# A high/low split of q and k moved to GpSimd, and x's low product moved to VectorE

## The chip, the cores and the metric

The kernel runs on one core of one Trainium2 chip. The time is device microseconds (us) of one execution; the time before is the median of 3 runs. The engines are PE (TensorE; its weight loads are shown as PEld), DVE (VectorE), ACT (ScalarE), POOL (GpSimd) and SP (SyncE, which here only issues DMAs).

## The reference, cut to what matters

Three stages follow one another: causal attention with a cumulative bias, a feed-forward layer with `h - tanh(h)`, and a second feed-forward layer with softmax weighting and a layer norm.

```python
scores = scale * q @ k.T                       # q, k: (4, 8, 576, 64), float32
cum = np.cumsum(np.maximum(s, 0.0), axis=-1)
scores = np.where(causal, -1e9, scores + np.minimum(-(cum[..., :, None] - cum[..., None, :]), 0.0))
attn = softmax(scores)
x = (attn @ v)                                 # -> (2304, 512)
h = x @ w_in;   x = (h - np.tanh(h)) @ w_out   # 512 -> 2048 -> 512
h = x @ w2_in;  ...                            # 512 -> 1024, solu, layer norm, -> 512
```

The change touches the attention stage alone.

## The kernel before, in words

**High and low parts.** TensorE's operands here have the type float32r. Each operand is held as two float32r parts, high (a converted copy) and low (the operand minus its high part), and a product is made of three: high with high, high with low, low with high. Every operand that comes out of PSUM therefore takes two passes: ScalarE writes the high part with a Copy from PSUM, and VectorE reads the same PSUM bank again, subtracts the high part and writes the low part.

**Pairs and slots.** The 32 heads are taken as 16 pairs of heads. The attention stage is a software pipeline of slots, numbered s = -1 to 17; `attention()` writes the first five and the last four out and runs slots 4 to 13 in a loop, two at a time. In slot s each engine works on several pairs at once, through closures that look up `sl.pair(k)`:

- k = 1, the pair s+1: its q and k are turned by TensorE (transposes with an identity) and split. `turn_qk(n)` (L1299 to L1302) turns part n into PSUM: n = 0 is the 64-row tail of k and q (192 columns), n = 1 the 512 columns of q, n = 2 the 512 columns of k. All three use one bank, `qk_ps`, so each must be read out before the next is turned. ScalarE's `qk_copy(n)` (L717) writes the high part and VectorE's `qk_rest(n)` (L994) the low part; `turn_qk(n)` waits for `qk_lo`, that is for VectorE, before it writes the bank again.
- k = 0, the pair s: scores (`score`, L1211 and L1215 for the mask; `score_tail`, L1229, L1231), VectorE's `bias` (L963, which also gives the row's maximum), ScalarE's `exp` (L707). The first matmul of `score(0, 1)` waits until all parts of q and k of this pair are split. GpSimd's `sums` (L537, L540) copies the tail's cumulative sums, and `split_v` (L568, L570) splits v into high and low.
- k = -1, the pair s-1: its probabilities are turned in seven units A01, A2, A3, T, B01, B2, B3 (`turn_p`, L1283), read out by ScalarE (`p_hi`, L698) and VectorE (`p_lo`, L946) in that order. The units share two banks in turn, so that TensorE writes a unit only when the unit two before it has its low part. `turn_rden` (L1311) and `rden_rows_copy` (L725) turn the reciprocal denominators; SP then writes them to memory and later reads them back, spread over the partitions. `attend(-1, 0, ...)` (L1254) multiplies the first head's probabilities with v.
- k = -2, the pair s-2: `attend(-2, 1, ...)` does the second head. One attend gives high products in 64 partitions of PSUM and low products in the other 64. ScalarE's `x_low_part(h)` (L732) copies the low product to the partitions of the high one, in SBUF; VectorE's `x_add(h)` (L976) adds the two into `x_sum`; GpSimd's `scale_x` (L557) multiplies with the reciprocal denominators into `xT`. `x_low_part(0)` and `x_add(0)` stand at the start of a slot, `x_low_part(1)` and `x_add(1)` in its middle.

**What sets the order.** Each engine runs its own instruction list in the order written at the end of its `slot` function; engines meet only at counting semaphores. TensorE's list in a slot is: score(0, 1), A01, A2, turn_qk(0), score(2), attend(-2, 1, 0), A3, turn_rden, the rest of attend(-2, 1), T, turn_qk(1), score(3), B01, B2, turn_qk(2), attend(-1, 0, 0), score_tail, attend(-1, 0, 1), B3, the rest of attend(-1, 0). SP's list is, too, one queue: in a slot it loads the next cumulative sums and v, then waits for `rden_rows`, writes the denominators out, and only behind that loads q and k of the pair s+2, whose parts `turn_qk` of the next slot needs.

From slot 15 on the first layer's work is woven in: `first_x` (L637 on ScalarE, L887 on VectorE) and `first_w1i` split x and weights, `first_up` is its matmuls.

Of the kernel before, what the change touches and what calls it, by code (L numbers as in the profile page):

```python
# [14 lines left out]
P = 128  # L15
# [35 lines left out]
def build_transformer(nc, q, k, v, s, w_in, w_out, w2_in, w2_out, g_ln, out):  # L51
# [59 lines left out]
    with ctx:  # L111
# [12 lines left out]
        with ExitStack() as phase:  # L124
            sb = tensors(phase, attention_words)
            qkT_hi = [sb(f"qkT_hi{n}", [P, QK_W], F32R) for n in range(2)]
            qkT_lo = [sb(f"qkT_lo{n}", [P, QK_W], F32R) for n in range(2)]
            probs = [sb(f"probs{n}", [P, PW]) for n in range(2)]
            pT_hi = sb("pT_hi", [P, 2, PT_W], F32R)

            v_parts = [sb(f"v_parts{n}", [P, NT, 4 * D], F32R) for n in range(2)]
            ident_b = sb("ident_b", [P, P], BF16)
            mask_b = sb("mask_b", [P, P], BF16)
            upper_b = sb("upper_b", [P, TAIL], BF16)
            lower_b = sb("lower_b", [P, TAIL], BF16)
            tail_mask_b = sb("tail_mask_b", [P, TAIL], BF16)
            neg_max = [sb(f"neg_max{n}", [P, TILES]) for n in range(2)]
            row_sum = [sb(f"row_sum{n}", [P, TILES]) for n in range(2)]
            den = [sb(f"den{n}", [P, TILES]) for n in range(2)]
            rden = [sb(f"rden{n}", [P, TILES]) for n in range(2)]  # L140
            rden_row = sb("rden_row", [TILES, P])

            w1i_words = GATE_W + FT * 2 * DM
            sb("gap", [P, w1i_words - sum(attention_words)])
            cum_bc = [sb(f"cum_bc{n}", [P, 2, S]) for n in range(2)]
            cum_tail = sb("cum_tail", [P, S])
            v_raw = [sb(f"v_raw{n}", [P, NT, 2 * D]) for n in range(2)]
            pT_lo = sb("pT_lo", [P, 2, PT_W], F32R)
            rden_T = [sb(f"rden_T{n}", [P, S]) for n in range(2)]
            x_low = sb("x_low", [P, S])  # L150
            x_sum = sb("x_sum", [P, S])
# [96 lines left out]
        cum_copied = sem("cum_copied")  # L248
        qk_hi = sem("qk_hi")
# [248 lines left out]
        def _(pool):  # L498
# [28 lines left out]
            def slot(sl):  # L527
                def sums():

                    if sl.runs(0):  # L530
                        pair, half, par = sl.pair(0)
                        pool.wait_ge(cum_in[par], 16 * (half + 1))
                        wait(pool, biased, TILES * pair)
                        wait(pool, v_split, 2 * pair)
                        wait(pool, x_done, pair - 2)
                        met(pool)
                        pool.tensor_copy(cum_tail[0:TAIL, :], cum_bc[par][0:TAIL, 0, :]).then_inc(cum_copied, 1)  # L537
                        pool.wait_ge(cum_copied, 2 * pair + 1)
                        met(pool)
                        pool.tensor_copy(cum_tail[TAIL:P, :], cum_bc[par][TAIL:P, 1, :]).then_inc(cum_copied, 1)  # L540

                def scale_x():
                    if sl.runs(-2):
# [7 lines left out]
                        if sl.runs(0):  # L551
                            pool.wait_ge(cum_copied, 2 * sl.pair(0)[0] + 2)
                        else:
                            pool.wait_ge(x_done, pair)
# [4 lines left out]
                def split_v():  # L559
                    if sl.runs(0):  # L560
# [3 lines left out]
                        pool.wait_ge(cum_copied, 2 * pair + 2)  # L564
                        wait(pool, x_done, pair - 1)
# [3 lines left out]
                        pool.wait_ge(v_split, 2 * pair + 1)  # L569
                        pool.tensor_tensor(low(v_parts[par]), raw, high(v_parts[par]).bitcast(F32),  # L570
                                           ALU.subtract).then_inc(v_split, 1)

                sums()
                scale_x()
# [50 lines left out]
        def _(act):  # L625
# [65 lines left out]
            def slot(sl):  # L691
# [19 lines left out]
                def qk_copy(n):  # L711

                    if sl.runs(1):
# [3 lines left out]
                        act.activation(qkT_hi[par][:, at:at + width], qk_bank(sl, n)[:, 0:width], ACT.Copy).then_inc(qk_hi, 1)  # L717
# [8 lines left out]

                def x_low_part(h):

                    if sl.runs(-2):
                        pair, half, par = sl.pair(-2)  # L730
                        act.wait_ge(attended, 2 * pair + h + 1)
                        act.activation(x_low[h * D:(h + 1) * D, :], x_ps[(1 - h) * D:(2 - h) * D, :],  # L732
                                       ACT.Copy).then_inc(x_low_done, 1)
# [14 lines left out]
                x_low_part(0)  # L748
# [10 lines left out]
                p_hi("A3")  # L759
                rden_rows_copy()  # L760
# [6 lines left out]
                x_low_part(1)  # L767
                p_hi("T")
                first_w1i(sl, 1)
                qk_copy(1)  # L770
# [5 lines left out]
                qk_copy(2)  # L776
# [88 lines left out]
        def _(dve):  # L865
# [73 lines left out]
            def slot(sl):  # L939
# [28 lines left out]

                def x_add(h):
# [18 lines left out]
                def qk_rest(n):  # L988

                    if sl.runs(1):  # L990
                        pair, half, par = sl.pair(1)
                        at, width = QK_PART[n]
                        dve.wait_ge(qk_hi, 3 * pair + n + 1)
# [3 lines left out]
                if sl.fixed and sl.s == 0:  # L997
# [12 lines left out]
                    return  # L1010
                bias(0, 0)
# [10 lines left out]
                qk_rest(0)  # L1022
# [3 lines left out]
                if sl.fixed and sl.s == LAST:  # L1026
                    step(0, 0)
                x_add(1)
                p_lo("T")
                first_w1i(sl, 1)  # L1030
                qk_rest(1)
# [5 lines left out]
                qk_rest(2)  # L1037
# [100 lines left out]
        def _(pe):  # L1138
# [58 lines left out]
            def slot(sl):  # L1197
# [88 lines left out]
                def turn_qk(n):  # L1286

                    if sl.runs(1):
# [6 lines left out]
                        else:  # L1295
                            wait(pe, qk_lo, 3 * pair + n)
# [31 lines left out]
                turn_p("A3")  # L1328
                turn_rden()
                attend(-2, 1, 1, 2, 3, 4)  # L1330
                turn_p("T")
                turn_qk(1)
# [5 lines left out]
                turn_qk(2)  # L1338
# [104 lines left out]
```

## Time and profile before

| what | us |
|---|---|
| median of 3 runs (lowest to highest) | 840.17 (839.23 to 841.72) |
| the profiled execution | 841.88 |
| its span, from the first to the last instruction | 840.1 |
| attention, slots -1 to 17 | about 0 to 232 |
| one slot of the loop, from one first bias to the next (120.65 to 133.13) | 12.48 |

The granted TensorE clock is 0.996 of full speed over the span. Busy shares over the whole span are PE 98%, DVE 54%, ACT 47%, POOL 15%, but the last three are averages over stages with different limits; in the attention stage VectorE and ScalarE are busy more than nine tenths of a slot. In the rows, a duration contains the time in which an instruction's end overlaps the next one's start: what an instruction takes from its engine is the distance from its start to the next start. A bracket at the end of a row gives how long the engine sat idle before it and who released it. In the chain of waits, "issue" is time in which the engine waited for nothing that the profile shows.

### The profile page before, as it was taken

Reading aid. Unit: us, or ns where it says so; the run is one execution under the profiler, and the core shown is the slowest. Engines: PE = TensorE matmul, PEld = TensorE weight load, DVE = VectorE, ACT = ScalarE, POOL = GpSimd, SP = SyncE. Lnnn points to the kernel's source line nnn. Section 1 sums busy time; section 2 is a strip of 40 time slices with the busy share of each in tenths; the row PEclk is TensorE's granted clock in tenths of the full one; section 3 lists DMA queues with packets and bytes.
Section 4 is the critical chain, followed back from the end, with each engine's and each line's share of the span. In section 5 each row is a group of like instructions: output and inputs, shape, how many; then the busy total and the mean of one; then the engine's idle time right before and its main releaser. Section 6 shows DMA issues by size and latency. Waiting matters only on the chain.

```text
span 840.1 us, 14119 instructions
## 1 busy us (share of the span) xinstructions
PE 821.1 (98%) x4552; PEld 706.4 (84%) x4552; DVE 452.4 (54%) x1059; ACT 395.1 (47%) x888; POOL 126.6 (15%) x150
## 2 busy tenths in 40 slices
PE   7999999998999999999999999999999999999998
PEld 6787787787888888888888888899988888888886
DVE  5889999988764342223223322333647554555452
ACT  4999999998744332223222322324533433333323
POOL 3334334334100000000000000000022212221110
PEclk9999999999999999999999999999999999999999
DMA  7454554554343200000000000000200100000001
GB/s 179 130 152 121 149 154 127 142 155 132 90 158 106 76 0 1 1 1 0 0 0 0 0 0 0 0 1 26 76 0 2 38 12 25 25 25 12 25 25 38
DMA packets 77714, 46.29 MB, mean 55 GB/s; under 512 B 59824, under 2 KB 68144, under 8 KB 77680
## 3 DMA queue, kind: packets, MB, share of 16 engines
q1 hardware_dynamic: 75232, 45.19, 18.9%
q10 hardware_dynamic: 2448, 0.66, 0.4%
q8 instruction: 19, 0.31, 0.2%
q14 instruction: 15, 0.12, 0.0%
HBM read 40.97 MB, written 4.87 MB: 55 GB/s over the span
## 4 chain that ended last, share of the span: by engine, by line
PE 82%; DVE 6%; issue 5%; ACT 4%; SPq 1%; DMA 1%; DVEq 0%; ACTq 0%
PE psum L1156 24%; PE psum L1169 24%; PE psum L1367 12%; PE psum L1395 11%; PE psum L1254 4%; ACT probs L707 2%; PE psum L1381 2%; PE psum L1211 2%; DVE pT_lo L946 2%; PE psum L1229 1%; PE psum L1283 1%; ACT x_low L732 1%; PE psum L1299 1%; DVE qkT_lo L994 1%; DVE probs L963 1%
## 5 line engine op out<-in xcount | busy, mean ns | idle before, releaser
L1156 PE MATMUL psum<-x_hi,w1i 128*128 128x464 f32 (+1 forms) x640 | 185.7, 371 | 0.4 <-DVE w1i L892 0.4
L1169 PE MATMUL psum<-gate_hi,w1o 128*128 128x464 f32 (+1 forms) x640 | 146.5, 371 | 0.0
L1156 PEld LDWEIGHTS psum<-x_hi,w1i 128*128 128x128 f32 x640 | 119.8, 188 | 14.8 <-DVE w1i L892 0.8
L1169 PEld LDWEIGHTS psum<-gate_hi,w1o 128*128 128x128 f32 x640 | 120.1, 188 | 13.6
L926 DVE TENSOR_TENSOR gate_lo<-gate,gate_hi 128x464 fp32r<-128x464 f32 (+1 forms) x80 | 51.1, 639 | 135.8 <-ACT gate_hi L677 135.8
L1156 PE MATMUL psum<-x_lo,w1i 128*128 128x464 f32 (+1 forms) x320 | 118.8, 371 | 0.0
L677 ACT ACTIVATE gate_hi<-gate 128x464 fp32r<-128x464 f32 (+1 forms) x80 | 47.1, 589 | 144.7 <-PE psum L1169 137.8
L916 DVE TENSOR_TENSOR gate<-psum,gate 128x464 f32<-128x464 f32 (+1 forms) x80 | 50.9, 636 | 97.3 <-ACT gate L666 97.2
L666 ACT ACTIVATE gate<-psum 128x464 f32<-128x464 f32 (+1 forms) x80 | 44.2, 553 | 107.2 <-PE psum L1156 104.5
L1395 PE MATMUL psum<-w2o,lnT_hi 128*128 128x512 f32 x288 | 91.8, 400 | 0.5 <-DVE lnT_lo L1112 0.5
L707 ACT ACTIVATE probs<-probs,neg_max 128x128 f32<-128x128 f32 (+2 forms) x144 | 83.7, 582 | 13.6 <-DVE neg_max L963 13.0
L1169 PE MATMUL psum<-gate_lo,w1o 128*128 128x464 f32 (+1 forms) x320 | 80.0, 371 | 0.0
L1367 PE MATMUL psum<-w2i,y_hi 128*128 128x512 f32 x288 | 77.4, 391 | 0.0
L946 DVE TENSOR_TENSOR pT_lo<-psum,pT_hi 128x512 fp32r<-128x512 f32 (+3 forms) x160 | 72.1, 479 | 4.1 <-ACT pT_hi L698 3.5
L698 ACT ACTIVATE pT_hi<-psum 128x512 fp32r<-128x512 f32 (+3 forms) x160 | 64.2, 437 | 11.2 <-PE psum L1283 9.2
L591 POOL CAST y_hi<-xT 128x512 fp32r (+1 forms) x18 | 11.0, 612 | 387.6 <-PE psum L1156 384.2
L963 DVE CUSTOM_DVE_ANT_0 probs<-psum,cum_bc 128x128 f32<-128x128 f32 (+3 forms) x128 | 58.8, 482 | 16.5 <-PE psum L1215 12.4
L1156 PEld LDWEIGHTS psum<-x_lo,w1i 128*128 128x128 f32 x320 | 60.1, 188 | 6.7
L1169 PEld LDWEIGHTS psum<-gate_lo,w1o 128*128 128x128 f32 x320 | 60.1, 188 | 6.5
L1283 PE MATMUL psum<-ident,probs 128*128 128x128 f32 x400 | 61.2, 278 | 3.0 <-DVE pT_lo L946 1.6
L1367 PEld LDWEIGHTS psum<-w2i,y_hi 128*128 128x128 f32 x288 | 54.0, 188 | 11.8 <-issue 0.2
L1395 PEld LDWEIGHTS psum<-w2o,lnT_hi 128*128 128x128 f32 x288 | 52.9, 189 | 11.9 <-issue 1.0
(109 smaller groups left out, 1226.0 us busy)
## 6 DMA issues: line engine op xcount, KB each, us to landing
cum_bc<-cum_dram SPq DMA_DIRECT2D x16, 576.0 KB, 5.0
rden_T<-rden_dram SPq DMA_DIRECT2D x32, 144.0 KB, 3.0
out_x<-out_sb SPq DMA_DIRECT2D x18, 256.0 KB, 2.0
stage<-in_q SPq DMA_DIRECT2D x32, 128.0 KB, 2.3
v_raw<-in_v SPq DMA_DIRECT2D x32, 128.0 KB, 3.6
stage<-in_moe_w_in SPq DMA_DIRECT2D x16, 256.0 KB, 3.0
stage<-in_moe_w_out SPq DMA_DIRECT2D x16, 256.0 KB, 3.1
stage<-in_k SPq DMA_DIRECT2D x28, 128.0 KB, 2.4
```

The lines of the kernel that those rows point to most:

```text
L677: act.activation(gate_hi[j % 2][:, 0:wide(c)], gate[j % 2][:, 0:wide(c)], ACT.Copy).then_inc(gate_hi_done, 1)
L698: hi = act.activation(to(pT_hi), ps, ACT.Copy)
L707: act.activation(probs[par][:, at:at + width], probs[par][:, at:at + width], ACT.Exp, bias=neg_max[par][:, col:col + 1], scale=-1.0, accum ...
L916: dve.tensor_tensor(gate[j % 2][:, 0:n], h_ps[j % 4][:, 0:n], gate[j % 2][:, 0:n], ALU.subtract).then_inc(gate_done, 1)
L926: dve.tensor_tensor(gate_lo[j % 2][:, 0:n], gate[j % 2][:, 0:n], gate_hi[j % 2][:, 0:n].bitcast(F32), ALU.subtract).then_inc(gate_lo_done, 1)
L946: lo = dve.tensor_tensor(to(pT_lo), ps, to(pT_hi).bitcast(F32), ALU.subtract)
L963: dve.tensor_tensor_reduce(probs[par][:, at:at + width], tail_bank(sl) if h is None else score_ps[h][t], cum_tail[:, :] if h is None else ...
L1156: mm = pe.matmul(h_ps[j % 4][:, 0:wide(c)], wp[j][:, kt, :], xp[:, kt, 0:wide(c)], start=(n == 0), stop=(n == 3 * KT - 1))
L1169: mm = pe.matmul(y_ps[m][:, 0:wide(c)], wp[j][:, m * P:(m + 1) * P], gp[j % 2][:, 0:wide(c)], start=(j == 0 and wp is w1o_hi and gp is gat ...
L1283: mm = pe.transpose(ps[:, n * P:(n + 1) * P], probs[par][:, at:at + P], ident[:, :])
L1367: mm = pe.matmul(h2_ps[par][:, half * BANK:(half + 1) * BANK], yp[par][:, kt, :], wp[kt][:, 4 * half:4 * half + 4, :].rearrange("q f p -> ...
L1395: mm = pe.matmul(out_ps[par], lp[par][:, f, :], wp[f][:, :], start=(f == 0 and n == 0), stop=(f == FT2 - 1 and n == 2))
```

## The change

Splitting q and k: for pairs 2 to 15 ScalarE's `qk_copy(n)` now writes a plain float32 copy of the turned part into one of two new SBUF buffers, `qk_flat[n % 2]`, and signals `qk_copied`. GpSimd's new `split_qk(n)` makes both parts from that buffer, a cast for the high and a subtraction for the low part. VectorE's `qk_rest` is left only for pairs 0 and 1 (slots -1 and 0). `turn_qk(n)` on TensorE now waits for ScalarE's copy, not for the low part. ScalarE's `qk_copy(0)` and `qk_copy(2)` wait for GpSimd to be done with the buffer that they reuse.

The low product of x: `x_low_part(h)` is a VectorE copy in place of a ScalarE one; its second half also waits for `rden_rows` of the slot.

Order: TensorE's `turn_qk(1)` moves ahead of `turn_rden` and of the rest of attend(-2, 1), `turn_qk(2)` moves from behind B2 to behind T; `qk_copy(1)` and `qk_copy(2)` move up on ScalarE in the same way. On GpSimd `split_qk` 0 to 2 stand between `sums` and `scale_x`.

```diff
+            qk_flat = [sb(f"qk_flat{n}", [P, FULL * P]) for n in range(2)]
...
@@ GpSimd
-                        wait(pool, x_done, pair - 2)
...
+                def split_qk(n):
+
+                    if sl.runs(1) and not (sl.fixed and sl.s <= 0):
+                        pair, half, par = sl.pair(1)
+                        at, width = QK_PART[n]
+                        flat = qk_flat[n % 2][:, 0:width]
+                        hi, lo = qkT_hi[par][:, at:at + width], qkT_lo[par][:, at:at + width]
+                        pool.wait_ge(qk_copied, 3 * pair + n + 1)
+                        if n == 0:
+                            pool.wait_ge(cum_copied, 2 * (pair - 1) + 2)
+                        else:
+                            pool.wait_ge(qk_lo, 3 * pair + n)
+                        met(pool)
+                        pool.tensor_copy(hi, flat).then_inc(qk_hi, 1)
+                        pool.wait_ge(qk_hi, 3 * (pair - 2) + n + 1)
+                        met(pool)
+                        pool.tensor_tensor(lo, flat, hi.bitcast(F32), ALU.subtract).then_inc(qk_lo, 1)
...
                 sums()
+                split_qk(0)
+                split_qk(1)
+                split_qk(2)
                 scale_x()
                 split_v()
...
@@ ScalarE
-                        act.activation(qkT_hi[par][:, at:at + width], qk_bank(sl, n)[:, 0:width], ACT.Copy).then_inc(qk_hi, 1)
+
+                        if sl.fixed and sl.s <= 0:
+                            to = qkT_hi[par][:, at:at + width]
+                        else:
+                            to = qk_flat[n % 2][:, 0:width]
+                            if n != 1:
+                                act.wait_ge(qk_lo, 3 * pair + (n == 2))
+                        act.activation(to, qk_bank(sl, n)[:, 0:width], ACT.Copy).then_inc(qk_copied, 1)
...
-                x_low_part(0)
...
                 p_hi("A3")
+                qk_copy(1)
                 rden_rows_copy()
                 exp(0, 2)
...
-                x_low_part(1)
                 p_hi("T")
                 first_w1i(sl, 1)
-                qk_copy(1)
+                qk_copy(2)
...
-                qk_copy(2)
...
@@ VectorE
+                def x_low_part(h):
+
+                    if sl.runs(-2):
+                        pair, half, par = sl.pair(-2)
+                        dve.wait_ge(attended, 2 * pair + h + 1)
+                        if h == 1 and sl.runs(-1):
+
+                            dve.wait_ge(rden_rows, pair + 2)
+                        dve.tensor_copy(x_low[h * D:(h + 1) * D, :], x_ps[(1 - h) * D:(2 - h) * D, :]).then_inc(x_low_done, 1)
...
+                x_low_part(0)
                 bias(0, 0)
                 bias(0, 1)
                 x_add(0)
...
-                qk_rest(0)
...
+                x_low_part(1)
                 x_add(1)
                 p_lo("T")
                 first_w1i(sl, 1)
-                qk_rest(1)
...
-                qk_rest(2)
...
@@ TensorE
-                            wait(pe, qk_lo, 3 * pair + n)
+                            wait(pe, qk_copied, 3 * pair + n)
...
                 turn_p("A3")
+                turn_qk(1)
                 turn_rden()
                 attend(-2, 1, 1, 2, 3, 4)
                 turn_p("T")
-                turn_qk(1)
+                turn_qk(2)
...
                 turn_p("B01")
                 turn_p("B2")
-                turn_qk(2)
                 attend(-1, 0, 0)
```

## Rows read from the trace of the kernel before

**Rows 1.** Busy time by stretch (PE, PEld, DVE, ACT, POOL), one slot of the loop

```profile
core 0: us, PE busy (x) PEld busy (x) DVE busy (x) ACT busy (x) POOL busy (x), PEclk, DMA share, GB/s
120.65:133.13 12.48, 12.30 (x102) 10.09 (x101) 11.45 (x35) 11.55 (x34) 5.03 (x5) 1.00 0.57 145
```

**Rows 2.** Chain of waits, same slot: start, us, what

```profile
120.65 0.11 DVE probs L963
...
122.75 0.04 ACT probs L707
...
127.28 0.69 DVE qkT_lo L994
...
128.02 0.66 PE psum L1299 x4
...
133.13 0.11 DVE probs L963
```

**Rows 3.** VectorE's timeline, same slot: start, duration, instruction

```profile
122.44 0.27 DVE L963 CUSTOM_DVE_ANT_0 probs<-psum,cum_bc 128x128 f32<-128x128 f32 x1
...
124.98 0.68 DVE L946 TENSOR_TENSOR pT_lo<-psum,pT_hi 128x512 fp32r<-128x512 f32 x1
125.88 0.76 DVE L976 TENSOR_TENSOR x_sum<-psum,x_low 64x576 f32<-64x576 f32 x1 [0.23 <-ACT x_low L732]
126.67 0.69 DVE L946 TENSOR_TENSOR pT_lo<-psum,pT_hi 128x512 fp32r<-128x512 f32 x1
...
131.22 1.21 DVE L946 TENSOR_TENSOR pT_lo<-psum,pT_hi 128x384 fp32r<-128x384 f32 x2
```

**Rows 4.** ScalarE's timeline, same slot

```profile
123.64 0.30 ACT L717 ACTIVATE qkT_hi<-psum 128x192 fp32r<-128x192 f32 x1
...
124.33 0.25 ACT L725 ACTIVATE rden_row<-psum 9x128 f32<-9x128 f32 x1
```

**Rows 5.** TensorE's timeline, same slot (short matmuls overlap; x4 is four of them)

```profile
122.91 0.60 PE L1283 MATMUL psum<-ident,probs 128*128 128x128 f32 x4
...
123.48 0.45 PE L1254 MATMUL psum<-pT_hi,v_parts 128*128 128x448 f32 x1
...
124.52 0.28 PE L1254 MATMUL psum<-pT_lo,v_parts 128*128 128x64 f32 x1
124.63 0.66 PE L1283 MATMUL psum<-ident,probs 128*128 128x128 f32 x4
...
125.70 0.50 PE L1211 MATMUL psum<-qkT_hi 64*128 64x512 f32 x2
...
126.72 1.25 PE L1283 MATMUL psum<-ident,probs 128*128 128x128 f32 x7
...
128.43 0.56 PE L1254 MATMUL psum<-pT_hi,v_parts 128*128 128x128 f32 x2
```

**Rows 6.** Groups of instructions, whole span, shapes kept apart

```profile
L994 DVE TENSOR_TENSOR qkT_lo<-psum,qkT_hi 128x512 fp32r<-128x512 f32 x32 | 21.9, 686 | 1.1 <-ACT qkT_hi L717 0.7
...
L1049 DVE COPY xT<-psum 128x464 f32 x4 | 2.4, 636 | 3.2 <-PE psum L1169 3.2
```

**Rows 7.** Groups of GpSimd, whole span, shapes kept apart

```profile
L594 POOL TENSOR_TENSOR y_lo<-xT,y_hi 128x512 fp32r<-128x512 f32 x18 | 23.3, 1295 | 3.3 <-POOL y_hi L591 3.3
...
L591 POOL CAST y_hi<-xT 128x512 fp32r x14 | 8.6, 612 | 0.0
```

**Rows 8.** VectorE's timeline in slot 15, L887

```profile
200.01 0.64 DVE L887 TENSOR_TENSOR x_lo<-xT,x_hi 128x464 fp32r<-128x464 f32 x1
202.89 1.55 DVE L887 TENSOR_TENSOR x_lo<-xT,x_hi 128x464 fp32r<-128x464 f32 x1
```

**Rows 9.** GpSimd's timeline in slot 15

```profile
202.52 1.42 POOL L557 TENSOR_TENSOR xT<-x_sum,rden_T 128x576 f32<-128x576 f32 x1 [6.84 <-DVE x_sum L976]
```

**Rows 10.** SP's queue, the slot of rows 1: start, issue time

```profile
130.52 0.65 SPq L395 DMA_DIRECT2D stage<-in_k  x1
```

**Rows 11.** DMA view, the same slot: last column us from issue to landing

```profile
stage<-in_k SPq DMA_DIRECT2D x1, 32.0 KB, 2.2
```

More of the change, by code:

```diff
@@ L248, in build_transformer @@
         cum_copied = sem("cum_copied")
+        qk_copied = sem("qk_copied")
         qk_hi = sem("qk_hi")
@@ L550, in scale_x @@
                         pool.wait_ge(rden_in[par], 32 * (half + 1))
-                        if sl.runs(0):
+                        if sl.runs(1):
+                            pool.wait_ge(qk_lo, 3 * sl.pair(1)[0] + 3)
+                        elif sl.runs(0):
                             pool.wait_ge(cum_copied, 2 * sl.pair(0)[0] + 2)
@@ L564, in split_v @@
                         pool.wait_ge(cum_copied, 2 * pair + 2)
+                        if sl.runs(1) and not (sl.fixed and sl.s <= 0):
+                            pool.wait_ge(qk_lo, 3 * sl.pair(1)[0] + 3)
                         wait(pool, x_done, pair - 1)
@@ L569, in split_v @@
                         pool.wait_ge(v_split, 2 * pair + 1)
+                        met(pool)
                         pool.tensor_tensor(low(v_parts[par]), raw, high(v_parts[par]).bitcast(F32),
@@ L725, in rden_rows_copy @@
                         act.activation(rden_row[:, :], rden_ps, ACT.Copy).then_inc(rden_rows, 1)
[L727 to L733, printed above, removed]
                 if sl.fixed and sl.s == 0:
@@ L992, in qk_rest @@
                         at, width = QK_PART[n]
-                        dve.wait_ge(qk_hi, 3 * pair + n + 1)
+                        dve.wait_ge(qk_copied, 3 * pair + n + 1)
                         dve.tensor_tensor(qkT_lo[par][:, at:at + width], qk_bank(sl, n)[:, 0:width],
@@ L1010, in slot @@
                     return
+                if sl.fixed and sl.s < 0:
+                    for n in range(3):
+                        qk_rest(n)
+                    return
+                x_low_part(0)
                 bias(0, 0)
```

## The prediction

> **What bounds the kernel now.** I began with the busy times of one slot [rows 1]. Of 12.48 us VectorE works 11.45 and ScalarE 11.55, GpSimd only 5.03: two engines are nearly full, and the one that gets work has room. A nearly full engine is no proof of a bound, so I read the chain of waits next [rows 2]. It closes in one slot: the slot's first bias at 120.65, a hand-over to ScalarE at 122.75, VectorE's low part of q at 127.28, which lets TensorE turn k at 128.02, and then TensorE alone up to the next first bias at 133.13. A slot is thus 7.37 us of alternating engines and 5.11 us of TensorE. Below, an offset is a time minus 120.65; the question is where the next first bias comes to lie.
>
> **What is removed and what is added.** VectorE loses three subtractions a slot: the two of 512 columns take 0.60 each from start to next start (686 ns with the overlap [rows 6]; p_lo(T), as wide, is followed after 0.61 [rows 2, 3]), the short one about 0.3. It gets two copies of 64x576 out of PSUM. No such copy is in the trace. Two rows bound it: VectorE's PSUM copy of 464 columns takes 636 ns [rows 6], and a 64x576 addition out of PSUM takes 0.76 [rows 3]. I take 0.75, and 0.64 and 0.76 as ends. So VectorE's load hardly changes (minus 1.5, plus 1.5). ScalarE loses two copies, and that is a real relief. GpSimd gets three casts and three subtractions: 512 columns cost 612 and 1295 ns [rows 7]; for the 192 columns I scale these down to an estimated 0.3 and 0.5. With an estimated 0.15 of waiting before each of the six this is about 5.5 us, so GpSimd stands at 10.5 to 11.7 of 12.5. It has no chain of its own: walked through, it begins when the first copy is there (offset 3.3), ends the last subtraction near 9.0, and the scores of the next slot need it at 11.1. The scaling of x and the split of v follow to about 13.3, and the sums and the next split fit before 15.9. I charge nothing for GpSimd; if that cover went, each us beyond two would lengthen the slot.
>
> **The early q turn.** Here the order matters. turn_qk(1) now stands behind A3. A3 starts at 122.91 [rows 5]; four transposes take 0.41 from start to next start (128.02 to 128.43 [rows 2, 5]), so TensorE comes to turn_qk(1) at offset 2.67. The bank is free when ScalarE has copied part 0, and that copy starts at 123.64 and takes 0.30 [rows 4]: offset 3.29, with the hand-over 3.37. Can the relieved ScalarE make it earlier? No: in front of it are two exps that begin at 122.75, released by VectorE's bias of 122.44 [rows 2, 3], and VectorE has no gap before that bias. So TensorE stands still for 0.70 in the place of shorter waits later.
>
> From 3.37 TensorE alone gives a lower bound. turn_qk(1) 0.41, the denominators 0.04 (estimated), the rest of attend(-2, 1) from 123.48 to 124.63, 1.15: T begins at 4.97. T 0.44 and turn_qk(2) with the change to the scores 0.57: score(3) at 5.98. score(3) from 125.70 to 126.72, 1.02: B01 at 7.00. Seven transposes at 0.11: attend(-1, 0, 0) at 7.77. From 128.43 to the next first bias are 4.70 [rows 2, 5]. Sum: 12.47, the slot of today.
>
> **The low product.** attend(-2, 1) ends 1.32 after its second part began (124.52 plus 0.28 minus 123.48 [rows 5]): at 3.82 plus 1.32, 5.14. VectorE is waiting by then, since even where it stands today p_lo(A3) ends at 5.01 [rows 3]. x_low_part(1) runs 5.18 to 5.93, x_add(1) 5.96 to 6.72, p_lo(T) 6.75 to 7.44. Today p_lo(T) ends at 6.71. B2 needs its bank: 7.49, so attend(-1, 0, 0) at 7.82 instead of 7.77, and TensorE's part ends at 12.52.
>
> x_low_part(0) stands at the end of the same stretch. The last p_lo (B3) ends at 132.43 [rows 3], 4.00 after attend(-1, 0, 0), because ScalarE must first read B3: here 11.82, and 0.05 later since ScalarE's exps are queued behind a later B01. x_low_part(0) runs 11.90 to 12.65 and the first bias begins at 12.68. VectorE, not the masks of TensorE, is then late, by 0.16. Slot: 12.68 against 12.48, plus 0.20.
>
> In this I let each of the four changes of partition wait for the instruction in front. The trace shows why: after x_add(1), on the upper 64 partitions, the next instruction starts 0.79 later, after its 0.76 have ended, whereas p_lo(T) is followed 0.61 after its start though it takes 0.69 [rows 3]. The Trainium skill (VectorE: DVE Perf Modes, "Two Vector instructions with no wait between them") says the same as a model: an instruction whose input or output starts in another quarter of the partitions than the last one's is held until all earlier ones have finished. By it both new copies and what follows them are held; without it the slot would be 12.5. The trace agrees with the rule.
>
> A second rule speaks against the change. In slot 15 a subtraction of 0.64 took 1.55 while GpSimd worked from 202.52 on [rows 8, 9]. Both its inputs are in SBUF. VectorE's instructions in slots 1 to 14 have one input in PSUM, and p_lo(T) or the subtraction at 127.28 are not longer beside GpSimd (0.69, 0.69) than p_lo(A3) without it (0.68 [rows 2, 3]). So I charge nothing. The Trainium skill (SBUF — State Buffer, "Who interferes with whom") draws this same line: only an instruction with two SBUF inputs, or in a two-port mode, contends with GpSimd. By the rule the cost is zero in these slots; the trace agrees.
>
> **The ends.** Slots 2 to 14 have both parts of the change: 13 times 0.20 is 2.6. Slot 1 has no x; by the same walk it loses about 0.3. Slot 15 splits no q and k, so VectorE only gets work: x_low_part(1) behind p_lo(A3) instead of beside it, about 0.55. Slots 16 and 17 hide most of it behind the first layer's matmuls; about 0.3 stays in the last one. Sum: 2.6 minus 0.3 plus 0.55 plus 0.3, about 3.1. The profiled execution took 841.88 (span 840.1 and 1.8 around it), so 845.0 by it; it was 1.71 above the median, so 843.3 against 840.17.
>
> **Rivals.** (a) No change: TensorE alone bounds the slot and the copies of x stay in its shadow. That is the 12.47 above; it holds if the holds or the 0.75 are smaller by 0.16 in all. With the ends, plus 0.5: 840.7. For it: the margin is small. Against: the row after x_add(1). 0.34.
> (b) Faster: ScalarE, relieved of its copies, has part 0 in SBUF by offset 2.67, and turn_qk(1) doesn't stand. Then TensorE's bound falls to 11.8, and VectorE's chain decides: x_low_part(1) at 5.04, p_lo(T) ends 7.30, slot 12.5 by rows and at best 12.25 with cheap copies. 13 times minus 0.23 plus 0.5 is minus 2.5 or better: 837.6. It decides only if the bias of 122.44 comes 0.6 earlier, for which I see no source. 0.13.
> (c) Slower by more: q and k arrive late. rden_rows_copy now stands behind qk_copy(1), which waits for the early turn: it starts at 4.50 instead of 3.68 [rows 4]. SP's loads are queued behind it. The last load of k is issued at 9.87 and lands 2.2 later, at 12.07 [rows 10, 11]; 0.8 later is 12.9, and turn_qk(0) wants it at 12.99. Nothing is left in reserve; if it comes 0.5 late in each slot, half of it behind the wait for the second bias, 3 to 4 us come on top: 847. 0.08.
> (d) The engines' contention does reach instructions with one SBUF input: then the 0.9 of slot 15 comes once or twice a slot, 13 to 25 us, 855 to 868. 0.03.
> My forecast, plus 3.1, has 0.42.
>
> **How the numbers follow.** A difference of 0.3%, 2.5 us, is about what a measurement of this kernel can tell from no change. The forecast's own range is 840.7 to 846 (a slot by 0 to 0.4 longer), and it holds the bound of 842.7, so a good part of it counts as no change. Same: 0.13 from the forecast, 0.27 from (a), 0.01 from (b), 0.41. Faster: 0.12 from (b), 0.02 from (a), 0.14. Slower: the rest, 0.45. The range goes from 837.6, which takes in the better half of (b), to 847.5, past (c), and leaves (d) out.
>
> **What would show it.** Right: VectorE's p_lo(T) at offset 6.75 and later; turn_qk(1) with some 0.6 idle in front, released by ScalarE's copy; x_low_part(1) waiting for TensorE; the first bias directly behind x_low_part(0) without a gap; no stall of the scores on GpSimd. Wrong: an idle VectorE before the first bias (then (a)); part 0 copied before 3.0 (then (b)); TensorE waiting for in_k (then (c)); subtractions on VectorE above 0.7 (then (d)).

## The result, and the profile after

The changed kernel took 844.33 us (median of 7 runs, 843.95 to 846.71) against 840.17 for the kernel before (7 runs, 839.23 to 841.95): ratio 1.0049, 95% interval 1.0034 to 1.0064. It is slower by half a per cent. The forecast was 843.3 and "slower" by a little.

I cut each profiled span at four places: the first bias of slot 2, the first bias of slot 15, the first matmul of the first layer that waits for w1i behind the attention stage ("first_up" in the tables), and the end. "Slots" is the distance between the first two, over 13.

| profile | slot 2 begins | slots 2 to 14, mean | slot 15 to first_up | rest |
|---|---|---|---|---|
| before | 32.61 | 12.567 | 36.08 | 608.04 |
| after | 31.95 | 12.762 | 39.02 | 608.02 |
| difference | -0.66 | +0.195 (x13 = 2.54) | +2.94 | -0.02 |

Now the slot of the loop that answers to rows 1 to 5. First the busy time by stretch, from one first bias to the next (PE, PEld, DVE, ACT, POOL):

```profile
121.25:134.00 12.75, 12.21 (x101) 10.12 (x100) 11.99 (x35) 10.35 (x33) 9.79 (x12) 1.00 0.55 139
```

Against [rows 1], ScalarE lost 1.2 us, GpSimd got 4.8 and VectorE is fuller than before: 11.99 of 12.75. Its own load was to stay the same. It rose by 0.5, and the timeline of VectorE shows where:

```profile
123.56 0.64 DVE L1018 TENSOR_SCALAR den<-row_sum 128x9 f32<-128x9 f32 x1
...
125.76 0.69 DVE L970 TENSOR_TENSOR pT_lo<-psum,pT_hi 128x512 fp32r<-128x512 f32 x1
126.48 0.75 DVE L1001 COPY x_low<-psum 64x576 f32<-64x576 f32 x1
127.27 0.76 DVE L1010 TENSOR_TENSOR x_sum<-psum,x_low 64x576 f32<-64x576 f32 x1
128.06 0.69 DVE L970 TENSOR_TENSOR pT_lo<-psum,pT_hi 128x512 fp32r<-128x512 f32 x1
...
132.49 0.69 DVE L970 TENSOR_TENSOR pT_lo<-psum,pT_hi 128x512 fp32r<-128x512 f32 x1 [0.22 <-ACT pT_hi L725]
133.21 0.76 DVE L1001 COPY x_low<-psum 64x576 f32<-64x576 f32 x1
134.00 0.29 DVE L987 CUSTOM_DVE_ANT_0 probs<-psum,cum_bc 128x128 f32<-128x128 f32 x1
```

The first row is the operation on the denominators, over 128x9 elements. It takes 0.64 here, and took 0.16 before, as the groups of instructions of the kernel before show:

```profile
L984 DVE TENSOR_SCALAR den<-row_sum 128x9 f32<-128x9 f32 x16 | 2.5, 159 | 0.0
```

One thing differs from the walk: x_low_part(1) doesn't wait for TensorE. It follows p_lo(A3) directly, since the longer operation makes VectorE late. The rest is as walked through: the copy takes 0.75; p_lo(T) starts 6.81 after the slot's first bias (6.75 was forecast); the last p_lo, the copy and the next first bias follow each other 0.72 and 0.79 apart, each start waiting for the end in front.

The chain of waits of the same slot:

```profile
121.25 0.14 DVE probs L987
...
124.31 0.22 ACT qk_flat L751
124.54 0.04 issue
124.58 0.66 PE psum L1336 x4
...
133.29 0.33 PE psum L1252 x4
133.62 0.35 PE psum L1320 x3
133.97 0.03 issue
134.00 0.29 DVE probs L987
```

turn_qk(1) is L1336: released by ScalarE's copy at offset 3.33 (3.37 was forecast). From there the chain as drawn runs on TensorE to the end. But the masks of the scores (L1252) are done at 133.62, while the first bias starts at 134.00, behind a VectorE copy that ends at 133.97. In the kernel xlow_scalar below, where no copy stands there, the bias follows 0.18 after the masks. So VectorE is late by about 0.20 (134.00 against 133.80); 0.16 was forecast.

TensorE's timeline has the stand before the early q turn. The bracket counts 0.50 from the end of A3; counted as I had counted, 0.41 behind A3's start, it is 0.69, and 0.70 was forecast:

```profile
123.48 0.60 PE L1320 MATMUL psum<-ident,probs 128*128 128x128 f32 x4
124.58 0.66 PE L1336 MATMUL psum<-ident,stage 128*128 128x128 f32 x4 [0.50 <-ACT qk_flat L751]
```

GpSimd's timeline, at the same time:

```profile
123.51 0.67 POOL L541 COPY cum_tail<-cum_bc 64x576 f32<-64x576 f32 x1 [0.16 <-POOL cum_tail L538]
124.77 0.34 POOL L556 CAST qkT_hi<-qk_flat 128x192 fp32r<-128x192 f32 x1 [0.60 <-ACT qk_flat L751]
125.30 0.60 POOL L559 TENSOR_TENSOR qkT_lo<-qk_flat,qkT_hi 128x192 fp32r<-128x192 f32 x1 [0.18 <-POOL qkT_hi L556]
...
129.10 1.29 POOL L559 TENSOR_TENSOR qkT_lo<-qk_flat,qkT_hi 128x512 fp32r<-128x512 f32 x1 [0.18 <-POOL qkT_hi L556]
131.03 1.42 POOL L578 TENSOR_TENSOR xT<-x_sum,rden_T 128x576 f32 x1 [0.64 <-POOL qkT_lo L559]
```

It waits for another engine once, 0.60 before the first cast; all its other gaps stand behind its own instructions. The last low part ends at offset 9.14, and the next slot's scores take it without a wait. So it is hidden, but without that one wait its queue would still need 12.1 us (12.75 less 0.60) for a slot.

The ends hold the surprise. The busy time by stretch of the changed kernel, in slot 16 (the column after the counts of GpSimd is the granted clock):

```profile
212.00:214.00 2.00, 0.85 (x6) 0.64 (x6) 1.94 (x4) 1.32 (x5) 0.00 (x0) 1.00 0.56 214
214.00:216.00 2.00, 1.88 (x8) 1.71 (x9) 1.97 (x8) 1.14 (x3) 0.00 (x0) 0.58 0.00 0
216.00:218.00 2.00, 2.00 (x11) 1.84 (x9) 1.19 (x2) 0.74 (x2) 0.00 (x0) 0.57 0.00 0
```

TensorE was busy 0.85 of the first 2 us, and then its granted clock fell to 1.2 GHz for most of the next 4, in which it had nothing but matmuls to do. From attend(-2, 1, 0) of slot 16 to the first layer's next matmul TensorE took 4.36, where it took 2.76 before at 2.4 GHz. That alone is 1.60 of the 2.94.

### The profile page after: what moved, and what is told of

The parts are those of the page before. It is cut to its first block, busy times and chain, and to the rows that moved or that the text cites. A ratio compares the mean times of both kernels' runs of the same rounds, so it can differ in the third digit from the quotient of the medians.

```text
span 844.9 us, 14328 instructions
## 1 busy us (share of the span) xinstructions
PE 820.2 (97%) x4552; PEld 707.7 (84%) x4552; DVE 461.7 (55%) x1049; ACT 375.6 (44%) x856; POOL 192.8 (23%) x234
## 4 chain that ended last, share of the span: by engine, by line
PE 84%; DVE 5%; issue 4%; ACT 3%; SPq 1%; DMA 1%; DVEq 0%; ACTq 0%
PE psum L1206 23%; PE psum L1193 23%; PE psum L1404 12%; PE psum L1432 11%; PE psum L1291 3%; PE psum L1320 3%; PE psum L1248 2%; PE psum L1418 2%; PE psum L1336 2%; DVE probs L987 1%; DVE pT_lo L970 1%; ACT pT_hi L725 1%; ACT probs L734 1%; PE psum L1266 1%; DVE x_low L1001 1%
```

## The experiments

All comparisons are against runs of the kernel before on the same chip (medians 840.57, 840.81 and 841.80 in the three sets of runs).

**The low product on VectorE, alone.** The kernel before with only `x_low_part` moved.

```diff
@@ ScalarE
-                x_low_part(0)
-                x_low_part(1)
@@ VectorE
+                x_low_part(0)
                 bias(0, 0)
...
+                x_low_part(1)
                 x_add(1)
```

> The kernel before with one part of the change: x_low_part on VectorE; q and k are split and turned as before. My theory (the two copies lie on VectorE's chain: p_lo(T) is pushed out by about 0.6, turn_qk(2) and attend(-1, 0, 0) follow it, and x_low_part(0) stands between the last p_lo and the first bias): a slot of 13.0 to 13.3 us against 12.57 on average before, 6 to 9 us in 13 slots, and the ends of the attention stage about 3 us longer as in the changed kernel; 849 to 852. Rival (VectorE's load is what counts, and 1.5 us fit in its gaps of 1.0 us): about 13.1 too, but with no idle time left on VectorE at all. Rival (the copies are hidden): 840.

850.37, ratio 1.0116 (1.0099 to 1.0133); slots 13.158. The two copies cost 0.59 a slot while VectorE still splits q and k. They stand on the chain of waits ("DVE x_low L967"). The relief for ScalarE does not make up for them.

**The split and the new order, without the copies.** The changed kernel with `x_low_part` back on ScalarE.

```diff
@@ VectorE
-                x_low_part(0)
-                x_low_part(1)
@@ ScalarE
+                x_low_part(0)
                 p_hi("A01")
...
+                x_low_part(1)
                 p_hi("T")
```

> The changed kernel with x_low_part back on ScalarE at its old places; GpSimd splits q and k, and the q and k turns stand early. My theory: the early turn of q still waits for ScalarE's first copy, so TensorE alone gives 12.5, and p_lo(T) still ends near 7.5 because x_low_part(1) comes late; without a copy before the first bias the slot is 12.50 to 12.60 (12.76 in the changed kernel), and the ends are as before: 839.5 to 840.5. Rival (GpSimd's work or its contention made the slot longer): it stays at 12.75, 842. Rival (the copies of x cost nothing in the slot): 12.75 too.

843.23, ratio 1.0028 (1.0018 to 1.0038); slots 12.717, seven of them 12.64 to 12.67; the longest are slot 2 with 12.88 and slot 5 with 12.87, in which TensorE also waits 0.79 for the load of k. My expectation missed by 3 us. The chain of this kernel measures TensorE alone:

```profile
123.31 0.32 ACT qk_flat L751
123.63 0.04 issue
123.68 0.66 PE psum L1334 x4
...
132.44 0.34 PE psum L1250 x4
132.84 0.13 issue
132.96 0.11 DVE probs L997
```

turn_qk(1) at offset 3.36, then 9.28 us of TensorE to the next first bias. I had summed 9.10 from distances between starts. So TensorE by itself gives 12.64, not 12.47 (12.55 by the changed kernel's masks, which end at 133.62, plus the same 0.18). Even without the copies the change lengthens the slot of 12.57. Rival (a) would have come out slower than I said.

**The old order of the turns.** The changed kernel, with `turn_qk(1)`, `turn_qk(2)` and the two ScalarE copies where they stood before.

```diff
                 turn_p("A3")
-                turn_qk(1)
                 turn_rden()
...
                 turn_p("T")
-                turn_qk(2)
+                turn_qk(1)
...
                 turn_p("B2")
+                turn_qk(2)
```

> The changed kernel with the old order of the turns (turn_qk(1) behind T, turn_qk(2) behind B2, ScalarE's copies with them); x_low_part stays on VectorE. If the early order is the fault, as 0.70 us of standing in front of turn_qk(1) may suggest: 12.5 or less, 840. My theory says otherwise: without the early turn attend(-2, 1) ends earlier, but VectorE reaches x_low_part(1) only at 5.2, p_lo(T) ends at 7.5 all the same, and now turn_qk(2) stands between B2 and attend(-1, 0, 0), 0.4 more; GpSimd gets part 2 later, and all it does moves towards the next slot: 13.0 to 13.3 a slot, 847 to 851.

853.91, ratio 1.0159 (1.0141 to 1.0176); slots 13.539, the later ones 13.65. That is 3 us slower than I expected. The early turns are not an extra: fed later, GpSimd ends its last low part late and the next scores wait for it, and TensorE's matmuls wait up to 0.7 for the denominators (its weight loads up to 1.0).

**The split alone.** GpSimd splits; the copies on ScalarE, the order as before (both edits above together).

> Only the split on GpSimd: x_low_part on ScalarE, all turns in the old order. VectorE has 1.5 us less to do and nothing more. My theory: p_lo(T) ends near 6.65, TensorE comes to attend(-1, 0, 0) at 7.45, a slot of 12.15 by TensorE; but part 2 reaches GpSimd only at about 8.7 and is ready near 11, so the scores of the next slot wait some tenths: 12.3 to 12.5, 836.5 to 839. Rival (GpSimd, with 12.1 us a slot in the changed kernel, becomes the bound and pushes itself on from slot to slot): 12.6 to 13, 841 to 846.

848.98, ratio 1.0095 (1.0074 to 1.0115); slots 13.158. I expected this one to be faster, and that theory fell. The rival came true in its effect, a longer slot, but not as it was put: GpSimd doesn't push itself on from slot to slot, since it still waits about 1.3 us in each for ScalarE's copies (0.96 and 0.32 in the slot shown). It is its delay that stands on the chain of waits:

```profile
119.10 0.50 ACT qk_flat L751
...
119.80 0.61 POOL qkT_hi L556
...
120.58 1.28 POOL qkT_lo L559
...
121.99 0.96 PE psum L1246 x12
...
125.87 0.88 DVE den L1018
```

k leaves PSUM at 119.1 to 119.6, and the first scores start 2.4 us later because cast and subtraction take 0.61 and 1.29 on GpSimd. And then the small operation on the denominators is on the chain with 0.88. Beside it, in the timelines of VectorE and GpSimd:

```profile
125.80 0.94 DVE L1018 TENSOR_SCALAR den<-row_sum 128x9 f32<-128x9 f32 x1
...
125.16 1.55 POOL L594 TENSOR_TENSOR v_parts<-v_raw,v_parts 128x640 fp32r<-128x640 f32 x1 [0.18 <-POOL v_parts L591]
```

It ends at 126.74, 0.03 after GpSimd's subtraction of v (126.71).

**The sums later.** The changed kernel with GpSimd's `sums()` behind `split_qk(0)`, and with the semaphore waits to match.

```diff
-                sums()
                 split_qk(0)
+                sums()
                 split_qk(1)
```

> The changed kernel with GpSimd's two copies of the sums behind the first split instead of in front of it, so that they no longer run while VectorE works on its small den operation. If GpSimd's work in SBUF holds that operation up (0.16 before, 0.61 to 0.64 after), it is back at 0.16 here. Then x_low_part(1) waits for TensorE as I had forecast, at an offset of 5.2, and the slot hardly gets shorter: 12.70 to 12.74, 843.7 to 844.3. A rival that takes this delay for the cause of the longer slot says 0.3 to 0.4 less a slot, 12.35 to 12.45 and 839 to 840.

844.71 (843.7 to 847.1), ratio 1.004 (1.0028 to 1.0051); slots 12.795, of which one is 13.11 and most are 12.74 to 12.77. The operation on the denominators met no copy of the sums any more, but in ten slots it met the subtraction of v and took 0.22 to 0.47 instead of the 0.16 that I expected; in the other three it took 0.16. x_low_part(1) waits for TensorE again (0.20). The slot stays: this delay, up to 0.5 us in ten slots of the changed kernel, costs nothing there, since x_low_part(1) has to wait for TensorE anyway. The changed kernel's own slots 4 and 7 say the same: there the operation took 0.16, and slot 7 is no shorter (12.74) than those around it.

**The low product left out.** The copies of x read and write the same partitions; the true low product isn't added. Everything else is as in the changed kernel.

```diff
-                        dve.tensor_copy(x_low[h * D:(h + 1) * D, :], x_ps[(1 - h) * D:(2 - h) * D, :])
+                        dve.tensor_copy(x_low[h * D:(h + 1) * D, :], x_ps[h * D:(h + 1) * D, :])
```

> The changed kernel, but x_low_part copies within the partitions in which the source lies (the high product in place of the low one), so that input and output start in the same partitions. It leaves out the low product of x. Everything else, the waits too, stays. If a change of partition holds the next instruction: what follows p_lo(B3), x_low_part(0) and p_lo(A3) starts about 0.08 before the end of the one in front in some of these places, 0.1 to 0.2 a slot in all; with TensorE's own chain at 12.64 the slot comes down to 12.64 to 12.68. Rival (the holds are nothing but waits on semaphores): no start changes, 12.75.

843.22 in its single run; slots 12.639, the steady ones 12.57. VectorE's timeline before a first bias:

```profile
131.59 0.69 DVE L970 TENSOR_TENSOR pT_lo<-psum,pT_hi 128x512 fp32r<-128x512 f32 x1 [0.21 <-ACT pT_hi L725]
132.20 0.74 DVE L1001 COPY x_low<-psum 64x576 f32<-64x576 f32 x1
132.91 0.29 DVE L987 CUSTOM_DVE_ANT_0 probs<-psum,cum_bc 128x128 f32<-128x128 f32 x1
```

The copy starts 0.61 after p_lo instead of 0.72, before that has ended, and the bias 0.71 after the copy instead of 0.79. The first change of partitions costs 0.11. The second costs at least 0.08, and how much more can't be seen, because the bias now stands 0.18 behind the masks and so is TensorE's again:

```profile
132.39 0.34 PE psum L1252 x4
```

Without them the slot is 0.12 to 0.17 shorter. The operation on the denominators takes 0.16 in nine slots of this run, which the run above shows to be worth nothing. The Trainium skill (VectorE: DVE Perf Modes, "Two Vector instructions with no wait between them") has as a rule that such an instruction starts only when every earlier one has finished; the runs agree.

**q and k loaded before the denominators.** In the changed kernel SP issues the loads of q and k ahead of its wait for `rden_rows`.

```diff
@@ SP, in the slot
+                if sl.runs(2) and not (sl.fixed and sl.s < 0):
+                    ...
+                    load_qk(pair, par)
                 if sl.runs(-1):
                     sp.wait_ge(rden_rows, pair + 1)
```

> The changed kernel with SP's queue turned round in a slot: q and k of the pair s+2 are loaded before SP waits for rden_rows. In the changed kernel TensorE waits 2.7 us in seven slots for in_k, and in more of them something unseen. My theory (VectorE decides the first bias, so these waits are taken up before score(2)): the waits for in_k vanish, the slot stays at 12.72 to 12.76, 844. Rival (the late loads of q and k are the cause of the longer slot): 12.6 or less, 842.

845.24, ratio 1.0049 (1.0034 to 1.0065); slots 12.756, as the changed kernel. TensorE's waits for in_k, 2.7 us in seven times in the changed kernel, are gone, and nothing is gained. Rival (c) came true as a wait and was worth nothing. The wait lies behind the first bias, before score(2), and something later in the slot takes it up; what does was not taken apart.

**The ends with the copies on ScalarE.** The changed kernel with `x_low_part` on ScalarE from slot 15 on.

```diff
@@ ScalarE
+                    if sl.runs(-2) and sl.fixed and sl.s >= PAIRS - 1:
@@ VectorE
-                    if sl.runs(-2):
+                    if sl.runs(-2) and not (sl.fixed and sl.s >= PAIRS - 1):
```

> The changed kernel, but in slots 15 to 17 x_low_part is on ScalarE again, as before; slots 2 to 14 are the changed ones. In the changed kernel the way from slot 15's first bias to the first full chunk of the first layer took 39.0 us against 36.1 before, 2.9 longer; 1.6 of these lie in slot 16, where the granted clock fell to 0.5 a second time behind TensorE's waits. My theory (VectorE's copies hold TensorE up in slots 15 and 16, and the waits bring the clock down): 36.2 to 36.6, no second stretch at half clock, 841.5 to 842 (844.3 changed). Rival (the second stretch is an accident of one profiled execution): it may be there again, and the time falls by 1 at most. Rival (the ends are paid by GpSimd's later work or later loads): 39 us as before, 844.

843.85 (842.3 to 846.26), ratio 1.0036 (1.0024 to 1.0047), 2 us above what I expected. The ends took 35.18, with the clock at 2.4 GHz throughout, but the start of this profile, with the same code, was 1.5 longer than that of the changed kernel (slot 2 begins at 33.42), with 6.8 us at 1.2 GHz in it instead of 3.4. The size of the ends' cost needed a fairer pair:

**Both kernels once more, unaltered.**

> The changed kernel once more, unaltered, for one profile: does TensorE's second stretch at half speed, during slot 16, come again? If it is bound to the changed kernel's work there, it stands again at 213 to 218 us and the way from slot 15's first bias to the end of slot 16 takes 39 us. If it hangs on small differences from run to run, it is gone and that way takes 36.5 to 37.5. The slots 2 to 14 give 12.74 to 12.78 either way.

> The kernel before once more, unaltered, for one profile, to price the way from slot 15's first bias to the end of slot 16 without the clock's part in it. With one stretch of 3.4 us at half speed it was 36.08. If the clock stays up here, 35.0 to 35.4, so that VectorE's copies of x cost 1.1 to 1.5 there (after_again: 36.50 with the clock up). If the same stretch comes again it is 36.0 to 36.2 and this comparison stays open but for ends_scalar (35.18). Slots 2 to 14 keep 12.57 on average.

844.50 and 841.47. In both the clock stays up through slots 15 and 16. The stretches of after_again that answer to those shown above:

```profile
212.00:214.00 2.00, 1.37 (x10) 1.12 (x10) 1.96 (x5) 1.48 (x5) 0.00 (x0) 1.00 0.68 259
214.00:216.00 2.00, 2.00 (x18) 1.94 (x17) 1.97 (x5) 1.19 (x3) 0.00 (x0) 1.00 0.03 12
216.00:218.00 2.00, 2.00 (x13) 1.81 (x12) 1.92 (x3) 1.12 (x2) 0.00 (x0) 1.00 0.01 2
```

| profile | slot 2 begins | slots 2 to 14, mean | slot 15 to first_up | rest |
|---|---|---|---|---|
| before_again | 33.20 | 12.566 | 35.07 | 608.07 |
| after_again | 32.17 | 12.766 | 36.50 | 608.07 |
| difference | -1.03 | +0.200 (x13 = 2.60) | +1.43 | 0.00 |

So of the 2.94 in the first pair 1.43 stays with the clock up, and 1.5 goes with the clock, which fell twice in the profile after and once in the one before (36.08 against 35.07). The 1.43 belongs to the copies of x, but for 0.11: ends_scalar, which has them back on ScalarE, takes 35.18, 0.11 more than before_again.

Laid over each other from slot 15's first bias on, TensorE's timelines of the two kernels show where it arises. TensorE is 0.66 late behind slot 15's x_low_part(1), 1.04 late at attend(-2, 1, 0) of slot 16, and 1.43 at the last point. In ends_scalar the three are 0.00, 0.12 and 0.11. The second place, in before_again and in after_again:

```profile
210.83 0.58 PE L1254 MATMUL psum<-pT_hi,v_parts 128*128 128x128 f32 x2 [0.35 <-DVE x_sum L976]
```

```profile
213.44 0.58 PE L1291 MATMUL psum<-pT_hi,v_parts 128*128 128x128 f32 x2 [0.63 <-DVE x_sum L1010]
```

**q alone on GpSimd.** The kernel before; ScalarE copies q plainly, GpSimd splits it behind `scale_x`; the tail and k stay with ScalarE and VectorE, and so do the copies of x and the order.

```diff
@@ GpSimd
                 scale_x()
+                split_q()
                 split_v()
@@ ScalarE, qk_copy
+                        if n == 1 and not (sl.fixed and sl.s <= 0):
+                            to = q_flat[:, :]
@@ VectorE, qk_rest
-                    if sl.runs(1):
+                    if sl.runs(1) and not (n == 1 and late):
@@ TensorE, turn_qk
+                        elif n == 2:
+                            wait(pe, qk_hi, 3 * pair + n)
```

> A version built from the readings: the kernel before, in which GpSimd splits part 1 alone, the 512 columns of q, from ScalarE's plain copy; parts 0 and 2 stay with ScalarE and VectorE, x_low_part stays on ScalarE, all turns stay in the old order; turn_qk(2) waits for the copy of part 1 instead of its low part. It takes 0.60 out of the one place where VectorE stood on the chain of waits (p_lo(T), then the low part of q, then turn_qk(2)), and gives GpSimd 2.2 us, placed behind scale_x so that VectorE's small den instruction isn't met. My theory: attend(-1, 0, 0) 0.3 earlier, a slot of 12.2 to 12.35 against 12.57, 836 to 838.5. Rival (ScalarE, busy 11.55 a slot, or TensorE is the next bound at once): 12.45 to 12.57, 839 to 840.5.

837.83 (10 runs, 837.44 to 840.09), ratio 0.997 (0.996 to 0.998); slots 12.348. Faster than both, at the weak end of what I expected. Its chain shows the next thing in line: TensorE waits for p_lo(T) before B2, and only behind that does it turn k.

```profile
123.77 0.70 DVE pT_lo L970
124.48 0.04 issue
124.52 0.55 PE psum L1309 x3
125.07 0.44 PE psum L1327 x4
```

**q alone, and k turned before B2.**

```diff
                 turn_p("B01")
+                turn_qk(2)
                 turn_p("B2")
-                turn_qk(2)
```

> The kernel q_alone (before, with the split of q alone on GpSimd) and k turned ahead of B2 on TensorE. In q_alone TensorE waits for VectorE's p_lo(T) before B2 (124.52 behind 123.77 and 0.70), and k's turn needs only ScalarE's copy. If that wait is the one that TensorE pays for, the turn of 0.4 us fills it: slot 12.0 to 12.2, 835 to 837. Rival: VectorE's queue sets the slot there, and k's bank being full earlier moves nothing: 12.35 and 837.8, or more if k's copy on ScalarE is now behind the exps of B01 and TensorE waits for it.

835.37 (834.55 to 835.62), ratio 0.9926 (0.9904 to 0.9947); slots 12.155, most 11.9 to 12.1, one of 13.07, in which TensorE waits 1.24 for the load of k. The turn fills the wait, and the chain is TensorE's own from the slot's second score to the next first bias:

```profile
124.36 0.44 PE psum L1309 x4
124.80 0.44 PE psum L1327 x4
125.24 0.33 PE psum L1309 x3
```

## Why the prediction was right, point by point

**The slot.** Plus 0.20 was forecast, and 0.195 and 0.200 were measured. The cause, VectorE's copy and its two changes of partition in front of the first bias, is shown: without the changes the steady slot is 12.57 (same_partitions), with them 12.74. But VectorE decides by less than the whole step. TensorE's own bound is 12.55 to 12.64 instead of 12.47: my sum came out 0.12 (in the changed kernel) to 0.18 short from turn_qk(1) to the next bias, in small pieces such as four transposes that took up to 0.52 to the next start where I had 0.41 and 0.04. Some luck is in the 0.20, too. I had started from one slot of 12.48, a short one, since the mean was 12.567. In the changed kernel the same slot takes 12.75, where I had forecast 12.68: there it is plus 0.27.

**The early q turn.** Right: released by ScalarE's copy of part 0, at offset 3.33. Rival (b) had no source for an earlier copy, and none appeared. The sign "x_low_part(1) waiting for TensorE" was seen in slots 2, 4 and 7 alone (0.48 to 0.52), the three in which the operation on the denominators took 0.16; in the others VectorE came to it too late to wait.

**The copy's price.** 0.75 forecast, 0.75 to 0.76 measured.

**GpSimd.** "I charge nothing" held for the changed kernel, and only with its order of turns. With the old order GpSimd's last cast and subtraction stand on the chain of waits: order_before gives 13.54 and split_alone 13.16, part of it from the denominators (see Contention). What I called cover is the early turn, and that is worth 0.78 a slot (13.54 against 12.76).

**Contention.** "VectorE's instructions in slots 1 to 14 have one input in PSUM" was wrong: the operation on the denominators reads and writes SBUF. It took 0.57 to 0.64 instead of 0.16 in ten of 13 slots of the changed kernel, and ended 0.02 to 0.03 after the GpSimd instruction beside it each time. I had left it out as too small to look at. It cost nothing here, because x_low_part(1) waits for TensorE behind it (sums_later), and it stood on the chain with 0.88 in split_alone. The p_lo subtractions of 512 columns, with one input in PSUM, took 690 ns on average in the slots 2 to 14, against 688 before, so rival (d) as put is refuted.

**The late loads, rival (c).** The waits came, and loads_first shows that they cost nothing in this kernel.

**The ends: the term that was mis-sized.** I had 0.55 plus 0.3 for slots 15 to 17. It is 1.43 with the clock up, and 2.94 in the profiled pair. The two places that I priced came out near: 0.66 in slot 15 and 0.39 at the last one. What was missing is slot 16, which I took to be hidden behind the first layer's matmuls. It adds 0.38, and 0.28 of that is the longer wait of attend(-2, 1, 0) for x_add(0) (0.63 against 0.35), which has the copy in front of it, on a VectorE that is nearly full (1.92 to 1.97 of every 2 us in the stretches of after_again above). And I did not ask what the clock does when TensorE waits longer.

**The start.** Minus 0.3 was forecast, minus 0.66 and minus 1.03 measured in the two pairs, but the runs don't show even the sign. The start goes with how long the clock was down. Up to slot 2's first bias xlow_vector runs the code of the kernel before and one copy of x more. It began slot 2 at 31.11 with the clock up, and the kernel before at 32.61 and 33.20, with 3.4 and 6.8 us at 1.2 GHz ahead of it. The changed kernel's code there began it at 31.95 and 32.17, and in ends_scalar at 33.42.

**The sum.** 2.6, minus 0.3, plus 0.85: 3.1. The second pair of profiles: 2.60, minus 1.03, plus 1.43: 3.0. The first pair: 4.8, of which the clock is 1.5. The medians differ by 4.2. Slots and ends alone, 2.60 plus 1.43, make 4.0, so the medians fit a start that is worth next to nothing (an estimate from these two figures). The forecast was 1.1 below the medians, 0.6 of it in the ends; that the second pair comes to 3.0 is luck.

## What to carry to other kernels

Do not move all instances of a work because the engine that has it is full: find the one that stands on the chain. Here one subtraction of three did. Moving it alone gave 0.3%, and reordering one turn behind it 0.3 to 0.4% more; moving all three and paying for them with copies on the same full engine lost 0.5%.

An idle engine that is slower per element is a delay before it is a load. GpSimd needs 1.9 us for both parts of 512 columns, one behind the other, where VectorE's low part took 0.69: a consumer must be at least that far away, or the producer must come earlier, as the early turns did. In split_alone GpSimd had idle time left in every slot, and the slot was 0.59 longer all the same.

After an edit, look at the instructions that you thought too small: the trace of after has them all, and one that grew from 0.16 to 0.64 points to a shared resource.

## What the runs showed of the hardware

VectorE's TENSOR_SCALAR of 128x9, SBUF to SBUF, alone takes 0.16 us. When a GpSimd instruction is already running it takes up to 0.96 and ends 0.02 to 0.04 us after that one's end: the copy of the sums ends at 124.18, the operation at 124.20; the subtraction of v at 126.71, the operation at 126.74. So it is held for the rest of the other's instruction and doesn't share. All cases fit one line: it ends at its start plus 0.16 or at GpSimd's end plus 0.03, whichever is later. In the changed kernel's slot 4, for one, it began at 59.80, 0.06 ahead of GpSimd's end, and took 0.16. Where it is not the later one to start, it isn't held. In slot 7 of the changed kernel both start at 98.09:

```profile
98.09 0.16 DVE L1018 TENSOR_SCALAR den<-row_sum 128x9 f32<-128x9 f32 x1
...
98.09 0.69 POOL L541 COPY cum_tail<-cum_bc 64x576 f32<-64x576 f32 x1 [0.16 <-POOL cum_tail L538]
```

In nine slots of same_partitions it starts 0.08 to 0.14 ahead of that copy, and takes 0.16. The Trainium skill (SBUF — State Buffer, "Who interferes with whom") says so: tensor_scalar is among the operations that can enter a mode with both of VectorE's port pairs, the second pair is shared with GpSimd, and whichever instruction issues first has it to its end. Here the runs agree on who is held and for how long; no row shows the mode. The prediction drew on this section, but didn't ask which small instruction could enter that mode.

TensorE's clock makes profiles of one kernel differ. In slots 15 and 16 the changed kernel had two stretches at 1.2 GHz in one profile and none in the other, and the kernel before one and none. Ahead of each fall TensorE had waited (in the changed kernel it was busy 0.48 of the 2 us from 204 and 0.85 of the 2 us from 212), but after_again waited nearly as long (0.49 from 204, 0.64 from 210) and its clock stayed up. So the waits are not enough to tell when it falls, and no run here settles what is. It is worth 39.02 against 36.50 for the same code: a difference of 2 us between two single profiles of this kernel proves nothing until the granted clock is compared stretch by stretch.
